# A block of matmuls on cleared memory ahead of TensorE's first work, in an attention, mixer and gated-convolution kernel

## The reference

```python
def _attn_ref(q, k, v, tau):                    # (4, 8, 576, 64) each
    scores = scale * np.matmul(q, k.transpose(0, 1, 3, 2))
    thresh = np.max(scores, axis=-1, keepdims=True) - tau
    scores = np.where(scores >= thresh, scores, -1000000000.0)
    scores = scores - np.max(scores, axis=-1, keepdims=True)
    attn = np.exp(scores)
    attn = attn / (np.sum(attn, axis=-1, keepdims=True) + 1e-09)
    return np.matmul(attn, v)

def _moe_ref(x, w_tok1, w_tok2, w_ch1, w_ch2):  # x (4, 576, 512)
    xt = x.transpose(0, 2, 1)
    h = np.maximum(xt @ w_tok1, 0.0) @ w_tok2
    u = x + h.transpose(0, 2, 1)
    return u + np.maximum(u @ w_ch1, 0.0) @ w_ch2

def _moe2_ref(x, w_in, conv_w, w_out):
    h = np.maximum(x @ w_in, 0.0)
    conv_out = three taps of conv_w along the sequence, applied to h
    gate = 1.0 / (1.0 + np.exp(-conv_out))
    return h * gate @ w_out
```

## Time and profile before

| | |
|---|---|
| time, median of 3 runs | 966.02 us (963.43 to 968.64) |
| span of the profiled execution | 967.4 us |
| TensorE busy | 941.2 us, 97% |
| VectorE, ScalarE, GpSimd busy | 492.5, 425.2, 371.7 us |
| DMA | 59.37 MB |
| mean granted TensorE clock over the span | 0.992 of 2.4 GHz |

### The profile page before, as it was taken

How to read it: one execution, slowest core, us unless ns; L and a number is a source line. 1 busy time by engine, 2 the same in 40 slices (tenths; PEclk the granted TensorE clock), 3 DMA queues, 4 the chain that set the end, 5 groups by cost and what they waited for, 6 DMA issues and landing times.

```text
span 967.4 us, 19928 instructions
## 1 busy us (share of the span) xinstructions
PE 941.2 (97%) x6896; PEld 894.9 (93%) x6896; DVE 492.5 (51%) x1134; ACT 425.2 (44%) x822; POOL 371.7 (38%) x284
## 2 busy tenths in 40 slices
PE   6799999999999999998999999999999999999998
PEld 5699999999999999997999999999999999989896
DVE  6657777777777777777221211212212281809190
ACT  4546656666666666653211201111102273727371
POOL 2445555545555455545511101011011572816361
PEclk9979999999999999999999999999999999999999
DMA  5863444434444434423200000000001001010101
GB/s 122 202 162 91 111 111 101 98 90 100 105 111 107 98 90 101 99 46 131 88 1 1 1 1 1 0 0 0 0 0 66 21 1 45 1 54 0 44 0 54
DMA packets 86590, 59.37 MB, mean 61 GB/s; under 512 B 67745, under 2 KB 68321, under 8 KB 86561
## 3 DMA queue, kind: packets, MB, share of 16 engines
q1 hardware_dynamic: 86560, 58.97, 24.5%
HBM read 26.36 MB, written 4.72 MB: 32 GB/s over the span
## 4 chain that ended last, share of the span: by engine, by line
PE 93%; SPq 3%; DMA 1%; POOL 1%; DVE 1%; ACT 0%; issue 0%; POOLq 0%; DVEq 0%
PE turn L1160 16%; PE pv L1055 12%; PE score L1238 11%; PE score L1160 10%; PE score L1020 9%; PE turn L1221 8%; PE turn L1037 7%; PE pv L1160 5%; PE turn L1092 4%; PE turn L1110 3%; PE pv L1221 2%; PE turn L1072 2%; PE turn L1008 2%; SPq L369 1%; PE pv L1062 1%; DMA qkT<-qk_hl 1%
## 5 line engine op out<-in xcount | busy, mean ns | idle before, releaser
L858 DVE SCALAR_TENSOR_TENSOR prob<-negs,thresh,exps 128x576 f32<-128x576 f32 (+1 forms) x160 | 156.4, 978 | 26.8 <-PE turn L1027 23.7
L833 DVE TENSOR_SCALAR_CACHE_REDUCE negs<-score 128x576 f32<-128x576 f32 (+1 forms) x160 | 120.5, 753 | 86.2 <-PE score L1020 82.9
L1020 PE MATMUL score<-qkT 128*128 128x288 f32 (+1 forms) x640 | 126.8, 321 | 10.5 <-DMA qkT<-qk_hl 10.5
L1055 PE MATMUL pv<-vn,probT 128*128 128x64 f32 x1024 | 132.1, 278 | 0.0
L645 ACT ACTIVATE exps<-negs,neg_max 128x576 f32<-128x576 f32 (+1 forms) x160 | 123.5, 772 | 11.5 <-DVE negs L833 11.4
L1055 PEld LDWEIGHTS pv<-vn,probT 128*128 128x128 f32 x1024 | 124.2, 195 | 3.2
L693 ACT ACTIVATE h3h<-score 128x288 fp32r<-128x288 f32 x64 | 26.3, 411 | 203.5 <-PE score L1160 203.5
L1020 PEld LDWEIGHTS score<-qkT 128*128 128x128 f32 (+1 forms) x640 | 90.7, 184 | 15.3 <-issue 6.6
L651 ACT ACTIVATE probT<-turn 128x512 f32<-128x512 f32 x128 | 75.9, 593 | 65.0 <-PE turn L1037 64.6
L551 POOL TENSOR_TENSOR ul<-uy,uh 128x1152 fp32r<-128x1152 f32 x7 | 18.7, 2674 | 206.9 <-ACT uh L687 206.9
L1037 PE MATMUL turn<-ident,prob 128*128 128x128 f32 (+1 forms) x640 | 92.7, 267 | 0.5 <-ACT probT L651 0.5
(11 more groups left out here) (161 smaller groups left out, 2318.7 us busy)
## 6 DMA issues: line engine op xcount, KB each, us to landing
qkT<-qk_hl SPq DMA_DIRECT2D x189, 144.0 KB, 2.6
qk<-in_q SPq DMA_DIRECT2D x32, 128.0 KB, 2.3
qk<-in_k SPq DMA_DIRECT2D x32, 128.0 KB, 2.5
vn<-in_v SPq DMA_DIRECT2D x32, 128.0 KB, 2.5
result<-ostage SPq DMA_DIRECT2D x16, 256.0 KB, 2.0
w1f<-in_moe_w_ch SPq DMA_DIRECT2D x4, 768.0 KB, 10.1
w2f<-in_moe_w_ch SPq DMA_DIRECT2D x4, 768.0 KB, 7.6
wif<-in_moe_w_in SPq DMA_DIRECT2D x1, 2048.0 KB, 7.8
```

The lines of the kernel that those rows point to most:

```text
L833: nc.vector.tensor_scalar(negs[0:w, t, :].rearrange("p (j c) -> p j c", j=2), score[slot][0:w, :, 0:HALF], -1.0, None, ALU.mult, ALU.min, ...
L858: nc.vector.scalar_tensor_tensor(out=prob[0:w, t, par, :], in0=negs[0:w, t, :], scalar=thresh[0:w, slot:slot + 1], in1=exps[0:w, slot, :], ...
L1020: mm = nc.tensor.matmul(score[slot][0:w, j, 0:HALF], qkT[:, par, 0, at:at + w], qkT[:, par, 1 + n, j * HALF:(j + 1) * HALF], start=(n == 0 ...
L1055: mm = nc.tensor.matmul(pvo[:, c, par, :], probT[:, kt, c * P:(c + 1) * P], vn[:, kt, par, 0:D], start=(par == 0 and c == 0 and kt == 0), ...
```

## The change

TensorE's list gets a function `warm_up()` in front of everything else. It waits until GpSimd has cleared two arrays, `zeros` (fp32) and `zeros_r` (fp32r), each 128 x 576, which lie on `uy`. Then it runs 12 matmuls of fp32r on half the rows with 288 columns (alternately on the upper and lower 64 rows, into two banks), 6 of fp32r on all rows with 128 columns, 6 of fp32 on all rows into half the output partitions with 256 columns (alternately the two halves), and 4 of fp32 on half the rows with 288 columns. It then waits for a second identity of type fp32r, and runs 4 transposes of 128 x 128 in fp32r and 8 transposes of fp32 on half the rows. No result is read.

GpSimd gets two memsets of 128 x 576 ahead of its others, and behind the identity one 128 x 128 copy of it into `ident_r`. Nothing is removed.

```diff
     ident = fixed.put("ident", [P, P])
+    ident_r = fixed.put("ident_r", [P, P], F32R)
...
+    zeros = nc.alloc_sbuf_tensor_at("zeros", [P, S], F32, offset=fixed.at - size([P, B, KM, S]))
+    zeros_r = nc.alloc_sbuf_tensor_at("zeros_r", [P, S], F32R, offset=fixed.at - size([P, KM, S]))
...
         @block.gpsimd
         def _(pool):
+            nc.gpsimd.memset(zeros[:, :], 0.0).then_inc(zeros_set, 1)
+            nc.gpsimd.memset(zeros_r[:, :].bitcast(F32), 0.0).then_inc(zeros_set, 1)
             nc.gpsimd.memset(vn[:, :, :, D:V1], 1.0).then_inc(cleared, 1)
...
                                     pattern=[[-1, P]], channel_multiplier=1).then_inc(ident_made, 1)
+            pool.wait_ge(ident_made, 1)
+            nc.gpsimd.tensor_scalar(ident_r[:, :], ident[:, :], 1.0, 1.0, ALU.mult, ALU.mult).then_inc(ident_made, 1)
...
+            def warm_up():
+
+                pe.wait_ge(zeros_set, 2)
+                for i in range(6):
+                    for r in range(2):
+                        rows = slice(r * D, (r + 1) * D)
+                        nc.tensor.matmul(banks[r][:, 0:HALF], zeros_r[rows, 0:P], zeros_r[rows, 0:HALF])
+                for i in range(6):
+                    nc.tensor.matmul(banks[2][:, 0:P], zeros_r[:, 0:P], zeros_r[:, 0:P])
+                for i in range(3):
+                    for r in range(2):
+                        to = slice(r * D, (r + 1) * D)
+                        nc.tensor.matmul(banks[3][to, 0:2 * P], zeros[:, to], zeros[:, 0:2 * P])
+                for i in range(2):
+                    for r in range(2):
+                        rows = slice(r * D, (r + 1) * D)
+                        nc.tensor.matmul(banks[r][:, 0:HALF], zeros[rows, 0:P], zeros[rows, 0:HALF])
+                pe.wait_ge(ident_made, 2)
+                for i in range(4):
+                    nc.tensor.transpose(banks[4][:, i * P:(i + 1) * P].bitcast(F32R), zeros[:, 0:P].bitcast(F32R), ident_r[:, :])
+                for i in range(4):
+                    for r in range(2):
+                        rows = slice(r * D, (r + 1) * D)
+                        nc.tensor.transpose(banks[r][:, i * D:(i + 1) * D], zeros[rows, 0:P], ident[rows, rows])
+
+            warm_up()
             pe.wait_ge(ident_made, 1)
```

More of the change, by code:

```diff
@@ L202, in build @@
         cleared = sem("cleared")
+        zeros_set = sem("zeros_set")
         set_once = sem("set_once")
```

## The result

The changed kernel takes 971.44 us (median of 18 runs, 968.32 to 974.92). The kernel before, in 18 runs of its own, takes 966.9 us (963.12 to 970.63). The ratio is 1.0046, with a 95% interval of 1.0035 to 1.0057: slower by 4.4 us (3.4 to 5.5), just inside the 0.5% that the prediction called no change.

A forecast was written before the change was run, and what follows sets the result against it. Bound: SP's list and transfers up to 49.33 us, set off by head 0's split. A 10.3 us slow-clock block, ending at 9.8 with the clock's rise, delays the drain 3.9 us: median 966.02 becomes 969.9, range 964.8 to 974.0.

The forecast's parts named there:

- What bounds the kernel up to the long wait: Up to 49.33 us: SP's list and its transfers are the bound, set off by the split of head 0.
- No gain from faster transposes of head 0: Head 0's transposes, 4.96 to 6.34 us: halving their time wins 0, as ScalarE's first drain waits for `tau` until 6.32.
- The terms of the block: Block from 1.9 us: per-group times, half-array matmuls taken as paired, sum 10.3 us at the slow clock, ends 6.0 and 17.5.
- The rise of the clock: In the block: TensorE goes to the fast clock 5.5 us after it starts, so the block ends at 9.8 us.
- The drain's lateness: ScalarE's first drain, head 0: starts at 10.2 us instead of 6.35, a delay of 3.9 us.
- One for one to the end: From head 0's split through SP's list to the end: the delay of 3.9 us passes on in full, without slack.
- The base of the sum: Whole kernel: profiled execution taken as 967.4 us, 1.4 us above the median of 966.02; with the delay 971.3.
- Score tiles on the fast clock from 15 us on: Score tiles from about 15 us: they should be at 0.13 to 0.16 us each.
- The long wait's end at 53.2: TensorE's long wait for SP's transfers: ends 3.9 us later than 49.33.
- half-array matmuls don't overlap: Rival, in the block: everything runs serially, 17.5 us of slow work, delay 7.5, median 973.5; chance 0.22.
- the delay is lost in the transfers: Rival, SP's transfers: the 10.86 us transfer lands at the same time; median 966 to 967; chance 0.22 shared with a short block.
- the block shifts the later slow stretch: Rival, 49.33 to 58.3 us: an earlier clock rise wins 1.75 us, no slow stretch 4.5; chance 0.08.

The follow-up runs named there:

- early `tau`: Kernel before, without a block, but tau loaded from ScalarE's queue instead of SP's: median 965.95 us, ratio 0.9993 to before.
- short block: Changed kernel with the block cut to its first 18 fp32r matmuls, no fp32 matmuls or transposes: median 966.16 us, ratio 0.9993 to before.
- twice: Changed kernel with `warm_up()` called two times in a row: median 976.63 us, ratio 1.0086 to the kernel before.
- one side: Changed kernel with all half-array matmuls on the same half, so none can run side by side: median 974.22 us, ratio 1.0074 to before.
- the wait without a block: Changed kernel without the block's matmuls; TensorE only waits while GpSimd clears a large array: median 972.14 us, ratio 1.0064 to before.
- the kernel with two filled waits: Kernel before plus tau early, one weight piece later, 8 matmuls in the long wait and 10 in the wait for GpSimd: 962.45 us, ratio 0.9950.

## Why the prediction held, point by point

- **What bounds the kernel up to the long wait: right.** SP's wait for head 0's split grew by what the drain was late, SP's list took 28.8 to 30.7 us from there in every kernel, and a lateness alone, without a block, cost at least as much as the block. That the idle time lies at the start is only partly so: 17 of before's 26 us are in the first 60, 5 lie between 430 and 470 and 4 at the very end. The change touches neither.
- **No gain from faster transposes of head 0, since `tau` holds the drain: right**, shown by the early `tau`, which moved the drain by 0.5 us, and by the short block, which won nothing.
- **The terms of the block.** From the starts of the rows after: 12 half-row fp32r matmuls 1.74 (forecast 1.7), 6 fp32r of 128 columns 1.47 (1.0, outside its bounds of 0.75 to 1.3), the 12 fp32 instructions 2.76 (2.7), the next 8 2.08 (2.0), the transposes 0.47 and 0.40 on the fast clock (0.4 and 0.6 there). The pairing, which no row of before showed, held and was shown by taking it away. For the 0.85 us of changes of shape there is no room: the starts leave at most 0.1 us beside each of the paired terms. At the slow clock the parts come to 9.8 us, where 10.3 was the sum: the term that was too small and those that were too large cancel, which is luck.
- **The rise of the clock: too early.** Forecast 5.5 us after the block's start, measured about 8 us in the changed kernel, 6 us in "twice" and 10 us in "one side". The 2.5 us more at half speed cost 1.25 us and, less the 0.25 us by which the sum was too large, put the block's end at 10.81 instead of 9.8. The term that was taken from a single rise of before is the one that had no firm value.
- **The drain's lateness**: 3.9 forecast, 5.0 measured. The first drain came 0.54 us after the block instead of 0.4. The rest is the line above.
- **One for one to the end**: right for the changed kernel, 4.4 of 5.0 us, with an interval of 3.4 to 5.5. For 9 us it may be 0.8. The median of 971.44 is 1.5 us above the 969.9 forecast: 0.9 us of that is the base, the median of three runs (966.02) where 18 give 966.9, and the rest is the larger lateness, less what was not passed on.
- **The base of the sum: wrong by 2 us, without effect.** I took the span of 967.4 for the execution's time. In all the runs since, the time is 1.75 to 2.25 us above the span, 2.1 as a rule, so that execution's time was about 969.4, one of before's slower ones; the median forecast of 969.9 came from adding the lateness to the median of the runs, and did not use it.
- **Score tiles on the fast clock from 15 us on: wrong.** The clock fell at 16.6, just behind the wait for `placed`, and rose at 20.0. It costs little if anything: TensorE waits for SP's transfers again at 24.23 (0.91 us), as in the kernel before.
- **The long wait's end at 53.2: not seen**, 50.59 in the profiled execution. The forecast took one execution's landing time of 10.86 us for the kernel's; it took 8.25 in the other, and the wait at this place ended at 46.2 to 49.3 in four kernels without a lateness, at 50.6 to 55.9 in the four with one. What I had named as a sign against the prediction (a late drain and an unmoved long wait) nearly came to pass in one pair of traces, while the other traces and 18 runs of each kernel say the opposite. The shift, not the absolute time, was what the forecast could give.
- **The rivals.** That half-array matmuls don't overlap fell by its own test. That the delay is lost in the transfers fell for most of it. That the block shifts the later slow stretch can't be excluded for a microsecond or two, but the wait without a block shows that it isn't needed.

## What to carry to other kernels

Filling to keep TensorE's clock is worth what the clock earns at that place, and only while it costs no lateness: read first what waits there anyway, how long, and what is on the path behind it. Here the start had half a microsecond of slack (the drain at 6.35 that could have been at 5.85) and nothing to gain, and the wait at 43 us had 3.6 to 6.4 us of slack and, in before's execution, 9 us of work at the lower level behind it. A clock raised ahead of a wait was lost again in all three kernels that had it (changed, "one side", "twice", each with a wait of 3.5 us): the filling belongs into the wait itself. With 2.9 us of it the clock held in five executions of twelve, with 4.7 us in eleven, and that much ran 1 us past the end of the wait. And where one trace of each kernel disagrees with many timed runs, look at the parts that vary from execution to execution (here one slow issue, one landing, and the length of the slow stretch) before believing the difference of two spans.

## What the hardware showed that I had not expected

- fp32r matmuls of 128 columns cost 0.245 us each at the lower level (1.47 us for 6), nearly the 0.28 of 288 columns, and 0.14 on the fast clock (0.82 us for 6 in the second block of "twice", from start to start), where four of 288 columns take 0.61 us, 0.15 each. Fewer columns saved little.
- The granted clock reads 1.00 until its first fall. It read 1.00 at 5 us in both kernels, while the durations show the lower level. The mean clock of the whole span is therefore lower where an early rise is followed by a fall: 0.9936 on average over 35 executions of before, 0.9906 over 18 of the changed kernel, though both spend their first score tiles at the lower level. The stretch from 16.6 to 20.0 alone is 0.0018 of the difference.
- The spread of this kernel's runs goes with the clock: over 35 executions of before, the span grows by 0.76 us for each 0.001 that the mean clock is lower (about two thirds of the variance), from 961.4 us at 0.996 to 969.2 at 0.987, and the six runs of the kernel with two filled waits spread over 1.4 us only. The work at the lower level behind the long wait lasted from 3.4 us (changed, "short block") to 16.8 us ("twice", 55.90 to 72.7) in the profiled executions.
